# A linear-attention and mixture kernel on one Trainium2 core: the opening of its first three chunks and the steps of the next three are put in another order

## What is computed

```python
for t in range(S):
    kt, vt, rt = (k[:, :, t], v[:, :, t], r[:, :, t])
    cur = np.einsum('bhd,bhe->bhde', u[None] * kt, vt)
    y[:, :, t] = np.einsum('bhd,bhde->bhe', rt, state + cur)
    state = w[None, :, :, None] * state + np.einsum('bhd,bhe->bhde', kt, vt)
x = attn_out.transpose(0, 2, 1, 3).reshape(B * S, H * D)      # 3072 x 384
h = x @ w_in                                                  # 384 x 2048
x = np.maximum(0.01 * h, h) @ w_out                           # 2048 x 384
# then: each token with x @ w_skip > 0 goes to one of 8 experts
# (argmax of x @ w_gate) and gets its relu(x @ w1) @ w2, times its gate, added
```

## Time and profile before

| what | us |
|---|---|
| median of 3 runs | 740.86 |
| lowest and highest | 736.67 and 741.08 |
| span of the profiled execution | 723.7 |
| TensorE busy in it | 689.5 (95%) |
| TensorE's mean granted clock | 0.981 of full |

### The profile page before, as it was taken

One profiled execution on the slowest core, in us unless ns is written; L12 is line 12 of the kernel. 1 busy time (PEld: TensorE's weight loads), 2 busy tenths in 40 slices (PEclk: granted clock), 3 DMA queues, 4 the chain that ended last, 5 costly groups with the idle time before them and its releaser, 6 DMA issues.

```text
span 723.7 us, 14127 instructions
## 1 busy us (share of the span) xinstructions
PE 689.5 (95%) x4365; PEld 650.8 (90%) x4366; DVE 404.6 (56%) x835; ACT 308.6 (43%) x664; POOL 106.4 (15%) x115
## 2 busy tenths in 40 slices
PE   8999999999999999999999999999998899998973
PEld 8899999999999999999999999999994688987773
DVE  7565665655646565556556555533557352745651
ACT  5354345333334433343444244333442453646630
POOL 5430000100010001001000100100102152443421
PEclk9799999999999999999999999999999999999997
DMA  8746624211422231242213222006015763383300
GB/s 229 233 129 194 195 67 126 73 42 33 129 63 67 90 88 31 60 129 67 67 44 99 64 59 88 12 12 240 1 44 213 260 232 139 112 285 139 101 19 8
DMA packets 38681, 77.44 MB, mean 107 GB/s; under 512 B 8568, under 2 KB 26902, under 8 KB 38624
## 3 DMA queue, kind: packets, MB, share of 16 engines
q1 hardware_dynamic: 33632, 62.37, 27.6%
q10 hardware_dynamic: 2432, 9.76, 4.1%
q0 software_dynamic: 2560, 4.58, 2.1%
HBM read 61.09 MB, written 12.41 MB: 102 GB/s over the span
## 4 chain that ended last, share of the span: by engine, by line
PE 82%; issue 4%; ACT 3%; DVE 3%; DMA 2%; POOL 2%; ACTq 1%; DVEq 1%; POOLq 0%; SPq 0%
PE bank L658 29%; PE bank L676 27%; PE bank L795 6%; PE bank L749 5%; PE bank L548 3%; PE bank L599 3%; PE bank L594 3%; PE bank L612 2%; PE bank L776 1%; ACT w_hi L1004 1%; PE bank L636 1%; DMA zg<-z_rows,id_get 1%; POOL kn L1485 1%; ACT am L850 1%; DVE h_sb L1154 1%
## 5 line engine op out<-in xcount | busy, mean ns | idle before, releaser
L889 ACT ACTIVATE h_sb<-bank 128x384 f32<-128x384 f32 x128 | 62.9, 491 | 249.8 <-PE bank L658 245.0
L1154 DVE TENSOR_TENSOR h_sb<-h_sb,bank 128x384 f32<-128x384 f32 x128 | 70.8, 553 | 174.9 <-ACT h_sb L889 174.5
L658 PE MATMUL bank<-x_hi,win_hi 128*128 128x384 f32 x384 | 135.8, 354 | 1.3 <-DVE x_lo L1141 1.3
L676 PE MATMUL bank<-wout_hi,g_hi 128*128 128x394 f32 x384 | 132.0, 344 | 0.0
L676 PE MATMUL bank<-wout_hi,g_lo 128*128 128x394 f32 x384 | 131.8, 343 | 0.0
L676 PE MATMUL bank<-wout_lo,g_hi 128*128 128x394 f32 x384 | 131.6, 343 | 0.0
L658 PE MATMUL bank<-x_hi,win_lo 128*128 128x384 f32 x384 | 130.5, 340 | 0.0
L658 PE MATMUL bank<-x_lo,win_hi 128*128 128x384 f32 x384 | 130.4, 340 | 0.0
L1507 POOL DMA_INDIRECT id_list<-idgate,dst x24 | 24.2, 1007 | 478.2 <-DVE dst L1252 473.4
L1161 DVE TENSOR_TENSOR g_lo<-h_sb,g_hi 128x384 fp32r<-128x384 f32 x128 | 71.8, 561 | 32.2 <-ACT g_hi L896 31.3
L896 ACT ACTIVATE g_hi<-h_sb 128x384 fp32r<-128x384 f32 x128 | 66.7, 521 | 43.4 <-DVE h_sb L1154 41.0
(11 more groups left out here) (180 smaller groups left out, 986.3 us busy)
## 6 DMA issues: line engine op xcount, KB each, us to landing
raw<-in_experts SPq DMA_DIRECT2D x32, 768.0 KB, 6.1
rkt<-in_rk_t SPq DMA_DIRECT2D x46, 192.0 KB, 3.9
rkn<-in_rk_nat SPq DMA_DIRECT2D x21, 384.0 KB, 4.4
v<-in_v_nat SPq DMA_DIRECT2D x24, 192.0 KB, 2.8
z_rows<-z_sb SPq DMA_DIRECT2D x24, 192.0 KB, 2.9
out<-z_sb SPq DMA_DIRECT2D x24, 192.0 KB, 2.9
stage<-in_win ACTq DMA_DIRECT2D x4, 768.0 KB, 5.9
stage<-in_wout_t ACTq DMA_DIRECT2D x4, 768.0 KB, 9.1
```

What stands on the lines that cost most here:

```text
L658: mm = pe.matmul(h_ps[t % 2][:, 0:GT], a[:, kk, cols], b[G % 2][:, kk, :], start=n == 0, stop=n == 3 * KT - 1)
L676: mm = pe.matmul(z_ps[i][:, 0:ZW], a[t % 3][:, tok], b[:, f, :], start=f == 0 and j == 0, stop=f == FT - 1 and j == 2)
L889: act.activation(h_sb[t % 2][:], h_ps[t % 2][:, 0:GT], ACT.Copy, scale=SLOPE).then_inc(s_h_scaled, 1)
L1154: dve.tensor_tensor(h_sb[t % 2][:], h_sb[t % 2][:], h_ps[t % 2][:, 0:GT], ALU.max).then_inc(s_leaky, 1)
```

## The change

- `multiply_rkt(n)` moves from POOL to VectorE and writes into `state[n]`. `am` is cleared in advance (POOL and VectorE), and POOL clears `state[n]` after `diagonals(n)`.
- `set_diag` is gone for chunks 0 to 2. In its place ACT's `diag_v(n)` makes eight products of v with the diagonal term, of 48 columns each, in `y_rows[n]`, and VectorE's `add_rows(n)` adds the bank of `outputs_rows(n)`.
- `w_k` is made right after the tables, `wk_turned` stands behind `diagonals(0)`, ACT copies `w_kn`.
- ACT issues `load_stage(0)` and `(1)` as soon as chunk 1's rows have landed; `load_rkt(3)` and `(4)` wait for the second of them.
- `state_sums(0)` to `(2)` move into the loop, behind `project(0)` and `project(1)`; their `update_state` to VectorE's steps 1 and 2. `scores(3)` still waits for all three.
- The first quarter of `win_lo` is made in four parts (`low_in_first`), the first gate products are cut in three pieces, and `load_stage(3)` waits for the fourth part.
- Chunks 3, 4, 5 begin at steps 2, 5, 8 (before 0, 4, 8).

```diff
-BEGIN = {CPG + i: 4 * i for i in range(CPG)}
+BEGIN = {CPG: 2, CPG + 1: 5, CPG + 2: 8}
...
-        y_rows = [sb2(f"y_rows{i}", [P, DM]) for i in range(2)]
+        y_rows = [sb2(f"y_rows{i}", [P, DM]) for i in range(CPG)]
...
+            def diag_v(n):
+
+                act.wait_ge(s_diag_cp, n + 1)
+                v_loaded(act, n)
+                for h in range(H):
+                    cols = slice(D * h, D * h + D)
+                    ins = act.activation(y_rows[n][:, cols], v_of(n)[:, cols], ACT.Copy,
+                                         scale=diag_of(n)[:, h:h + 1])
+                ins.then_inc(s_dv, 1)
...
+            def add_rows(n):
+
+                dve.wait_ge(s_y_done, n + 1)
+                dve.wait_ge(s_dv, n + 1)
+                dve.tensor_tensor(y_rows[n][:], rows_in_bank(n)[:, 0:DM], y_rows[n][:],
+                                  ALU.add).then_inc(s_y_out, 1)
...
             scores(0)
             diagonals(1)
             scores(1)
+            outputs_rows(0)
             diagonals(2)
-            outputs_rows(0)
             scores(2)
...
+            gate_products(0, (1, 2))
             hidden(0)
-            pe.wait_ge(s_gates_in, 16)
-            gate_products(0)
-            for n in range(CPG):
-                state_sums(n)
+            gate_products(0, (3,))
             hidden(1)
...
                 project(step)
+                if step == 0:
+                    state_sums(0)
+                    state_sums(1)
+                elif step == 1:
+                    state_sums(2)
...
             mask_scores(0)
+            multiply_rkt(1)
             scale_r(2)
             scale_k(2)
             mask_scores(1)
-            dve.wait_ge(s_y_done, 1)
-            dve.tensor_copy(y_rows[0][:], y_ps[:, 0:DM]).then_inc(s_y0_out, 1)
+            multiply_rkt(2)
+            add_rows(0)
             mask_scores(2)
+            add_rows(1)
             low_turned(0)
...
                 if n is not None and n < CHUNKS - B:
                     update_state(n)
+                if step == 1:
+                    update_state(0)
+                    update_state(1)
+                elif step == 2:
+                    update_state(2)
```

More of the change, by code:

```diff
@@ L933, in _ @@
             act.activation(spare[:], kn[0][:, 0, 0:1], ACT.Copy)
-            act.wait_ge(s_const_in, 16)
-            out_diag(0)
-            set_diag(0, range(H))
+            rkt_loaded(act, 1)
             load_stage(0)
-            out_diag(1)
-            set_diag(1, range(H))
             load_stage(1)
-            out_diag(2)
-            set_diag(2, range(H))
-            act.dma_start(const[:, 2 * P:], consts[:, 2 * P:]).then_inc(s_const2_in, 16)
-            load_stage(2)
-            high_in(0)
             act.wait_ge(s_tables_done, 1)
             act.activation(w_k[:], w_r[:, :, ::-1], ACT.Copy).then_inc(s_wk_done, 1)
-            act.wait_ge(s_y0_out, 1)
-            act.sem_inc(s_y_out, 1)
-            out_rows(1)
+            out_diag(0)
+            act.wait_ge(s_wkn_t, 1)
+            act.activation(w_kn[:].rearrange("a h d -> a (h d)"), y_ps[:], ACT.Copy).then_inc(s_wkn_done, 1)
+            diag_v(0)
+            out_diag(1)
+            load_stage(2)
+            diag_v(1)
+            out_diag(2)
+            act.dma_start(const[:, 2 * P:], consts[:, 2 * P:]).then_inc(s_const2_in, 16)
+            high_in(0)
+            diag_v(2)
             high_turned(0)
-            out_rows(2)
             high_turned(1)
             high_turned(2)
+            load_stage(3)
             high_out(0)
-            load_stage(3)
             scale_h(0)
@@ L961, in _ @@
             load_stage(5)
-            set_diag(3, range(H))
             scale_h(1)
             high_g(1)
+            set_diag(3, range(H))
             for step in range(STEPS):
@@ L1162, in low_g, with low_in_first @@
                                   ALU.subtract).then_inc(s_g_lo_done, 1)
+            def low_in_first(i):
+                cols = slice(P * i, P * i + P)
+                dve.wait_ge(s_win_hi, 1)
+                dve.tensor_tensor(win_lo[:, :, cols], stage[:, 0].rearrange("a (k c) -> a k c", c=512)[:, :, cols],
+                                  win_hi[:, :, cols].bitcast(F32), ALU.subtract).then_inc(s_win_lo, 1)
             def low_in(q):
@@ L1286, in _ @@
             mask_scores(1)
-            dve.wait_ge(s_y_done, 1)
-            dve.tensor_copy(y_rows[0][:], y_ps[:, 0:DM]).then_inc(s_y0_out, 1)
+            multiply_rkt(2)
+            add_rows(0)
             mask_scores(2)
+            add_rows(1)
             low_turned(0)
-            dve.wait_ge(s_wkn_t, 1)
-            dve.tensor_copy(w_kn[:].rearrange("a h d -> a (h d)"), h_ps[0][:]).then_inc(s_wkn_done, 1)
-            low_in(0)
+            low_in_first(0)
+            add_rows(2)
             low_turned(1)
             low_turned(2)
+            for i in range(1, 4):
+                low_in_first(i)
+            low_out(0)
+            leaky(0)
+            low_gates(0)
+            low_g(0)
             for q in range(2):
@@ L1313, in _ @@
             sum_diag(3)
-            for n in range(CPG):
-                update_state(n)
-            leaky(1)
-            low_g(1)
             for step in range(STEPS):
```

128 lines of the change are left out of this document (76 added, 52 removed).

## The result

| | before | after |
|---|---|---|
| median of four runs each, us | 738.76 | 759.23 |
| lowest and highest, us | 735.29 and 741.08 | 757.34 and 760.95 |
| profiled execution: time, span, us | not printed, 723.7 | 757.34, 755.6 |
| granted clock in it, of full | 0.981 | 0.953 |

The changed kernel is slower: the ratio is 1.0289, with an interval of 1.0235 to 1.0343. The ratios in this document leave out executions that lie more than 1.5% above the fastest one of their kernel, so they can differ from the quotient of two medians.

The account below looks back on a forecast made before the run. TensorE was taken to bound the loop, a chain over ACT, VectorE and DMAs the opening. Terms 4.2 + 2.2 + 1.1 + 4.7 + 3.4 = 15.6 on 740.9 gave 756.5, plus 1.0 for the clock: 757.5 us, range 746 to 765.

Parts of the forecast that it names:

- the waits in the loop: TensorE idle before scores(3), scores(4) and scores(5), released by VectorE's state updates: 4.9, 2.2 and 4.7 us.
- scores(6), and hidden(16) ...: 2.0 and 1.4, the least certain.: Loop, chunk 5's rows: y rows pass one x_sb in turn, each freed a step later, costing 2.0 and 1.4 us.
- hidden(8): 1.1: Loop: win's third part is issued some 5 us later, behind ACT's wait for outputs, costing hidden(8) 1.1 us.
- term one: Opening through scores(3): TensorE stands at 50.1 us against 45.95 before at the same work, +4.2 us.
- I add 1.0 for part of the clock's answer.: Whole kernel: 1.0 us added to the summed 756.5 for TensorE's clock falling, giving 757.5 us.
- each wait also drops the clock: Rival: half clock follows the two loop waits near 5 us and some smaller ones, +3 to +5, 760 us; 18 in 100.
- hidden(0) starts at about 28.4: End of the opening: the chain over VectorE and ACT lets hidden(0) start at 28.4 us, against 24.3 before.
- The ring turns: Opening, chunks 0 to 2: each turn is serial, mask 1.3, product 0.6, diagonals 1.0, scores 1.1 us.
- the chain of 19.4 us: From load_stage(3) at 29.6 us to update_state(2): serial ACT and VectorE work of 19.4 us, ending at 49.0.
- The median of the runs is 17.2 us above it, so I work out a shift of that span.: Baseline: the shift of the profiled 723.7 us span is added to the 740.86 us median.

Follow-up runs that it names:

- products early: Changed kernel with multiply_rkt(1) ahead of mask_scores(0) and multiply_rkt(2) ahead of scale_r(2): median 753.35 us; with the loop part undone as well, 736.95 us.
- loop undone: Changed kernel with its new opening but the loop of before (chunks 3, 4, 5 begin at steps 0, 4, 8): 741.31 us, ratio 1.0043 to before.
- idle filled: Changed kernel plus four wake-up products ahead of diagonals(0) and four unread products between scores(0) and diagonals(1): 754.15 us, ratio 1.0309 to before.

## Why the prediction was right, and where it was wrong

The forecast was 757.5 us, and the median is 759.23. The direction and the cause of the larger part, the waits in the loop, stand. Two of its steps failed, the price of the clock and the start of hidden(0). That the total is within 1.7 us is in part luck: the kernel before came out 2.1 us lower (738.76, not 740.86), so that a rise of 16.6 us was forecast and one of 20.5 measured.

- *The waits in the loop.* Confirmed, nearly to the tenth: scores(3) 4.98 us (4.9 foreseen), scores(4) 2.16 (2.2), scores(5) 4.67 (4.7), each released by update_state. At scores(3) the tenth is luck: TensorE came there at 55.1 us and the update ended at 60.1, both 11 us later than foreseen, and with the clock up in the opening (products early) the wait was 6.38. The experiments removed nearly all of them by the mechanisms named: the third update behind low_in(1), update_state one step late, and ACT's wait for outputs. The idle 3.1 and 8.3 us of set_diag were expected at 3 and 6.
- *"scores(6), and hidden(16) ...: 2.0 and 1.4, the least certain."* Oversized. The x_sb turn is on the chain of waits of the kernel after, piece by piece (L440; three of ten moves):

```profile
111.70 0.51 SPq L440
112.25 0.59 SPq L440
...
117.53 0.59 SPq L440
```

  but at its end hidden(16) waits 0.6 us for x_lo, and scores(6) for no state. TensorE, already late by the earlier waits, needed the rows later. The same holds for *hidden(8): 1.1*: nothing in the kernel after, and 0.96 as soon as the wait ahead of it is mended. In sum the waits foreseen were 16.3 us (4.9, 2.2, 1.1, 4.7, 2.0 and 1.4), of which term one took 4.2 for the first, and 12.4 us of idle time are there. Adding waits one behind the other can count a delay twice, where the first one already covers the second.
- *"I add 1.0 for part of the clock's answer."* Too little. Beside the waits the clock took 4.9 us of the same stretch (87.69 busy against 82.75), which is the rival's price of 3 to 5. The rival "each wait also drops the clock" was right for the two waits near 5 us, and should have been part of the forecast: 12.4 + 4.9 = 17.3 us for the loop, against 16.6 forecast for the whole change.
- *"hidden(0) starts at about 28.4."* Failed: 38.2. The ring turns were right in kind (diagonals(1) wait 2.0 us for product(1)), and diag_v took 1.90 us, as chosen. The step left out is that the clock can fall in the opening too, and for long; its price was laid on the waits of the loop alone. At half clock, TensorE's own products became the bound of the opening: the same opening (products early, in two kernels) ends at 27.6 us with the clock up and at 37.7 without. What made the clock fall is not shown. The waits that the ring brought come just before it in the changed kernel, but it fell as well with those waits filled (at 18.8 us) and with the products early (at 11.6). With the clock up, scores(3) came at 48.75, against 49.0 foreseen: the chain of 19.4 us was drawn about right, for a clock that the changed kernel's profile didn't have.
- *"The median of the runs is 17.2 us above it, so I work out a shift of that span."* This step hid the error. The kernel before runs at a lower mean clock in most executions than in the profiled ones, and that accounts for the gap in size: 13.3 us between 723.89 and 737.19, and an estimate of (0.984 - 0.966) x 735 = 13 us from the mean clocks of the two. If it loses the clock in its opening, as the changed kernel does, then the ten us that hidden(0) came late in the profile are mostly in both medians. This is argued, not shown; what is measured is that with the loop undone the whole new opening costs +0.4%. A forecast of the difference of spans would have been 16.6 against a measured 31.9, and of medians 16.6 against 20.5.

On diag_v, the Trainium skill (ScalarE: Activation LUTs, What ACT_TABLE_LOAD costs) gives an ACTIVATE 186 ns and 0.833 ns for each column, 93 ns more for a scale by partition, and 93 ns of overlap between two in a row. An estimate from that page is 8 x (186 + 93 + 40) - 7 x 93 ns, 1.90 us; the trace has 1.90.

On the clock, the rows show a fall after the idle time up to 15.9 us, then 30.70 us busy of 30.70 at 0.50, and the full clock again at 46.6 us, after hidden(0), hidden(1) and a part of hidden(2). The Trainium skill (TensorE: Matmul & The Clock Gate, What's actually happening) says that the idle engine falls to half clock and that work releases it. The fall behind idle time agrees in this kernel. The release doesn't, for those 30.7 us of unbroken work, and with the idle time filled the clock fell all the same, after 13.17 busy us of 13.80.

What stays open is why one execution of a kernel loses the clock in the opening and the next one doesn't. That the slower executions of the kernel before lose their time there is argued from their mean clock, since both of its profiles are at a high clock; it was not seen in a trace.

## What to carry to other kernels

In an in-order queue, a wait that is asked for one step too soon holds all that stands behind it (here 8.3 us of ACT, and a good part of the 4.67 us at scores(5)): place each wait on another engine behind the work that is ready, and take the distance between producer and consumer from the slowest queue, before chunks are packed closer. Before a profiled span is compared with a median, compare the granted clocks of the two; a gap between them may be the clock and not overhead. Where TensorE waits, price the wait and the half clock behind it together (here 12.4 us and 4.9), and allow for a lost clock in the opening as well (here ten us).

## What the runs showed of the hardware that was not expected

- TensorE's clock stayed at half for 30.7 us (15.9 to 46.6) while its records have no gap. In this stretch stand the diagonals, scores, outputs_rows, turns and gate_products; in two kernels with one and the same opening, its end came at 27.6 us with the clock up and at 37.7 with half clock from 11.6 us on. Unbroken work doesn't prevent the fall either: it came at 18.8 us after TensorE had been busy 13.17 of 13.80 us (idle filled).
- One kernel on one chip: 724.3 to 741.0 us for the kernel before in 29 executions, at a mean granted clock of 0.980 for the fastest and 0.959 and 0.962 for the two slowest. Four executions of the kernel with the products early differ by 12.4 us (746.14 to 758.52), at 0.971 and 0.951.
- Waits of 4.98 and 4.67 us cost more than themselves: the 12.4 us of idle time in that stretch came with 4.9 us of slower work, and with 13.7 us more at half clock than in the kernel without the waits.
